# The expert stage's token tiles are turned by VectorE in one operation each, and the second tile's inner rows by TensorE

## The chip, the cores and the metric

One core of one Trainium2 chip. The metric is the device time of one execution in microseconds; the figure compared is the median of several runs. Lower is better.

## What is computed

All arrays are float32. The input of the expert layer comes from a small attention between 8x512 tokens and 8x32 state rows; its 4352 output rows of 512 columns go through eight experts and then a dense two-layer block:

```python
xread = softmax(x @ state.T / 8) @ state
sread = softmax(state @ x.T / 8) @ x
t = concatenate([xread, sread])            # 4352 rows of 512, heads side by side
e = argmax(t @ w_gate)                      # one expert per row, E = 8
h = maximum(t[e == i] @ w1[i], 0)           # 512 -> 1024
y = gate_weight * sigmoid(...) * (h @ w2[i])    # 1024 -> 512
u = y @ w_in                                # 512 -> 2048
g = where(u >= 1, u, where(u <= -1, 0, (u + 1)**2 / 4))
out = g @ w_out                             # 2048 -> 512
```

## The kernel before

The kernel has three stages. Every engine's instructions are written out by hand, each engine in its own program, and semaphores tie them together.

**Stage one (0 to about 150 us).** Eight steps, one for each batch, do the attention. The rows that come out are scattered to DRAM (`slot_x`) by GpSimd, sorted by expert. SP's queue loads the tokens of the next steps and, between them, the four units of the first expert's weights. A short passage at its end (VectorE's `choose`, `find`, `best_expert`, then the tables of tiles) works out which 128 rows make which tile and which expert each tile has. In this passage tiles 0 and 1 are already loaded and turned (`first_x`, `first_xs`).

**Stage two, the expert tiles (about 150 to 590 us).** There are 38 tiles of 128 rows, in a loop over t. A product needs its left operand with the contraction dimension on the partitions, so each tile's 128x512 rows are turned to `KD` = 4 blocks of 128x128, and the 128x1024 inner rows to `K1` = 8 blocks. A float32 value is split into a high part (rounded to the fast type) and a low part (the rest), and each product is three matmuls: high by high, high by low, low by high. For tile t:

- TensorE: `up(t)`, 24 matmuls of 512 columns (L1620), gives the inner rows of tile t in `pC`. `turn_x(t + 1)`, 4 transposes against the identity (L1554), turns the next tile's rows. `down(t - 1)`, 24 matmuls (L1665), gives the output of the tile before. So TensorE runs one tile behind itself: it does `up` of one tile while VectorE turns the inner rows of another.
- ScalarE: `relu(t)` to `hrow` (L723), `x_hi(t + 1)` (L700), the load of tile t + 2 to `xtile` (L719), `y_out(t - 1)` (L735, and its store L738), `h_hi(t)` in two halves (L729).
- VectorE: `turn_h(t)`, 16 transposes of 32x256, which turn the inner rows (L1220); after the first four of them `x_lo(t + 1)` (L1073); at the end `h_lo(t)` in two halves (L1230). `down(t)` waits for `hlo_done`, which the last of them raises.
- GpSimd splits the weights of the experts to come (L476, L478), four units each, and scatters the rows' places (L551). SP's queue loads those units to `stage` (L365).

VectorE's transpose works inside blocks of 32x32: element (i, j) of a block goes to (j, i) of a block, and a block stays in its group of 32 partitions unless the instruction's output is in another group. `turn_h` therefore issues one instruction for each pair of groups, 16 in all.

The order of TensorE's round is this piece of its program:

```python
def turn(t):
    up(t)
    turn_x(t + 1)
    down(t - 1)
```

Tile 1 is special: its inner rows are turned by `turn(1)` on VectorE, while tile 0's are turned by TensorE (`turn_first_h`, L1676), since VectorE is still busy with the tables then.

**Stage three (about 590 us to the end).** Nine blocks of rows go through the dense layers, with `hidden` (L1716) and `result` (L1730) on TensorE. Rows of the first blocks are already weighed and turned beside the last tiles of stage two (`turn_y`, L1702).

Of the kernel before, what the change touches and what calls it, by code (L numbers as in the profile page):

```python
# [30 lines left out]
P = 128  # L31
# [4 lines left out]
def build(nc, x, state, w_gate, w_ogate, w1, w2, w_in, w_out, out):  # L36
# [42 lines left out]
    with ctx:  # L79
# [251 lines left out]
        def rows_of(t):  # L331
            return xtile[:, :] if t is None else first_x[t][:, :]

        def quarter(e, q):
            return e % 2 * 2 + q // 2
# [16 lines left out]
        def _(sp):  # L352
# [15 lines left out]
            def expert_unit(e, q):  # L368
                if q < 2:
                    k = UNIT // F1  # L370
                    return w1[bass.ds(e, 1), q * k * P:(q + 1) * k * P, :].rearrange("o (k p) n -> p (o k) n", p=P)
                k = UNIT // DM
                return w2[bass.ds(e, 1), (q - 2) * k * P:(q - 1) * k * P, :].rearrange("o (k p) n -> p (o k) n", p=P)

# [7 lines left out]
            for b in range(2, B):  # L382
                load_x_next(b, b % 2)
                if b == 2:
                    for q in range(2):
                        load_unit(expert_unit(0, q), q)
                if b in (B - 3, B - 2):
                    q = 2 if b == B - 3 else 3
                    sp.wait_ge(weights_split, q - 1)
                    load_unit(expert_unit(0, q), q % 2)  # L390

            def load_expert(e, units):
                for q in units:
                    sp.wait_ge(weights_split, 4 * e + q - 1)
                    load_unit(expert_unit(e, q), q % 2)
# [48 lines left out]
        def _(pool):  # L444
# [25 lines left out]
            def split_unit(e, q, unit):  # L470

                at = W[:, bass.ds(quarter(e, q), 1), :, (q % 2) * UNIT:(q % 2 + 1) * UNIT]
                hi = at[:, :, HI, :].rearrange("p o n -> p (o n)")
                lo = at[:, :, LO, :].rearrange("p o n -> p (o n)")
                pool.wait_ge(stage_loaded[q % 2], 16 * (2 * e + q // 2 + 1))
# [51 lines left out]
            shift(B - 1, 1)  # L527
            pool.wait_ge(tile_loaded, 32)
            scatter(B - 3, 1)
# [43 lines left out]
            def next_expert(e):  # L573
# [6 lines left out]
                with pool.If(end < start + 1):  # L580
                    for q in range(4):
                        pool.wait_ge(stage_loaded[q % 2], 16 * (2 * e + q // 2 + 1))
# [28 lines left out]
        def _(act):  # L611
# [13 lines left out]
            def split_first(m, q):  # L625

                act.wait_ge(stage_loaded[q], 16 * m)
                hi = W[:, bass.ds(m - 1, 1), HI, q * UNIT:(q + 1) * UNIT].rearrange("p o n -> p (o n)")
# [125 lines left out]
            wait_for_rows()  # L754
            act.dma_start(xtile[:, :], slot_x[bass.ds(row, P), :]).then_inc(tile_loaded, 16)
            act.wait_ge(logit_shifted, 1)
# [121 lines left out]
        def _(dve):  # L878
# [354 lines left out]

            def turn(t, reuse=True):
                turn_h(t, 0, 1, reuse)
                x_lo(t + 1)
                turn_h(t, 1, 4)
                h_lo(t)

            slots_of_rows()  # L1240
            logits_of_rows()
            dve.wait_ge(hhi_done, 2)
            nc.vector.tensor_tensor(first_hs[:, LO, :, :], pD[:, :].rearrange("p (k s) -> p k s", k=K1),
                                    first_hs[:, HI, :, :].bitcast(F32), ALU.subtract).then_inc(hlo_done, 1)
# [73 lines left out]
            for a in range(2):  # L1318
                y_lo(a, 0, a)
            turn(tail + 1)  # L1320
            for a in range(2, BIG):
# [26 lines left out]
        def _(pe):  # L1348
# [200 lines left out]

            def turn_x(t, place=None):  # L1550
                pe.wait_ge(tile_loaded, 16 * (t + 1) if place is None else 32)
                turned, _ = x_at(place)
                for k in range(KD):
                    last = nc.tensor.transpose(turned[:, k * P:(k + 1) * P], rows_of(place)[:, k * P:(k + 1) * P], ident[:, :])  # L1554
                last.then_inc(xt_made, 1)
# [5 lines left out]
            turn_x(0, place=0)  # L1561
            pe.wait_ge(prob2_done, b + 1)
# [27 lines left out]
            pe.wait_ge(pT_copied, b + 1)  # L1590
            turn_x(1, place=1)
            pe.wait_ge(slots_found, r + 1)
# [42 lines left out]
            def up_first_two():  # L1635
# [9 lines left out]
                for n in range(2):  # L1645
                    pe.wait_ge(relu_done if n else relu_begun, 1)
                    if n:
                        turn_first_h()
                    for i in range(3 * KD):
# [21 lines left out]

            def turn_first_h():
                pe.wait_ge(relu_done, 1)
                pe.wait_ge(xread_copied[0], 2 * (B - 1) + CH)
                for k in range(K1):
                    last = nc.tensor.transpose(pD[:, k * P:(k + 1) * P], first_hrow[:, k * P:(k + 1) * P], ident[:, :])  # L1676
                last.then_inc(ht_made, 2)
# [114 lines left out]
```

## Time and profile before

| | us |
|---|---|
| median of 3 runs (1345.02 to 1346.15) | 1345.86 |
| the profiled execution, device time | 1341.72 |
| its span in the trace | 1339.70 |
| TensorE busy | 1318.6 (98%) |
| VectorE busy | 935.5 (70%) |
| ScalarE busy | 409.7 (31%) |
| GpSimd busy | 386.7 (29%) |

The span is the time from the first to the last instruction of the profiled execution; the device time holds what lies around it too. TensorE's busy time is modelled from the pipelined matmuls, so it tells that there is always one under way, not that each is as short as it could be. The chain of waits goes back from the last instruction to whatever released each step; what stands on it set the end. The granted TensorE clock is 0.996 of full speed over the span.

### The profile page before, as it was taken

To read this page: it belongs to the slowest core of one execution; us is meant where nothing else is said; L and a number is where in the kernel's file an instruction comes from. 1 tells how busy PE (TensorE), PEld (TensorE's weight loads), DVE (VectorE), ACT (ScalarE), POOL (GpSimd) and SP (SyncE) were. 2 spreads that over 40 slices of the span, in tenths; PEclk is the share of its full clock that TensorE was granted. 3 is DMA by queue.
4 is the path that set the end of the run, shared out by engine and by line. 5 is a ranking of instruction groups with operands and counts; after the bars stand their busy time and mean duration, and the time that the engine had idled before them with its cause. 6 is when DMAs were issued, how large, how long until landed. Compare 5 with 4: busy or idle time off the path is not lost.

```text
span 1339.7 us, 20092 instructions
## 1 busy us (share of the span) xinstructions
PE 1318.6 (98%) x6518; PEld 1104.4 (82%) x6519; DVE 935.5 (70%) x2001; ACT 409.7 (31%) x641; POOL 386.7 (29%) x213
## 2 busy tenths in 40 slices
PE   8999999999999999999999999999999999999996
PEld 6999888888888888887888888888888888888885
DVE  3667888888888888867777576675775767757343
ACT  3466322222222222322222222222222222222232
POOL 2377473876580939470010100100101001010010
PEclk9999999999999999999999999999999999999999
DMA  6556343534442425530010100100100001010000
GB/s 151 163 167 219 121 110 114 166 111 139 141 146 73 141 86 197 159 103 16 16 40 17 40 16 16 39 16 8 39 18 37 16 16 39 16 40 1 0 32 16
DMA packets 80589, 100.57 MB, mean 75 GB/s; under 512 B 46112, under 2 KB 46112, under 8 KB 80032
## 3 DMA queue, kind: packets, MB, share of 16 engines
q1 hardware_dynamic: 60160, 61.94, 15.3%
q10 hardware_dynamic: 13856, 20.19, 5.2%
q0 software_dynamic: 6528, 17.87, 3.5%
q8 instruction: 24, 0.39, 0.1%
q14 instruction: 21, 0.17, 0.0%
HBM read 69.80 MB, written 30.18 MB: 75 GB/s over the span
## 4 chain that ended last, share of the span: by engine, by line
PE 95%; DMA 1%; DVE 1%; ACT 1%; SPq 1%; ACTq 0%; issue 0%; POOL 0%; POOLq 0%; DVEq 0%
PE area L1716 27%; PE area L1730 27%; PE area L1665 16%; PE area L1620 15%; PE area L1430 2%; PE area L1400 2%; PE area L1420 1%; PE area L1554 1%; DMA xin<-in_x 1%; PE area L1387 1%; SPq L347 1%; PE area L1447 1%; DMA st_diag<-in_state 0%; PE area L1454 0%; DVE yrow L1259 0%
## 5 line engine op out<-in xcount | busy, mean ns | idle before, releaser
L1730 PE MATMUL area<-W,gs 128*128 128x512 f32 x1632 | 394.1, 389 | 1.8 <-DVE gs L1304 1.8
L1716 PE MATMUL area<-ys,W 128*128 128x512 f32 (+1 forms) x1728 | 394.3, 377 | 0.0
L1716 PEld LDWEIGHTS area<-ys,W 128*128 128x128 f32 x1728 | 313.4, 188 | 61.2
L1730 PEld LDWEIGHTS area<-W,gs 128*128 128x128 f32 x1632 | 305.2, 188 | 65.2 <-DVE gs L1304 2.6
L1220 DVE STREAM_TRANSPOSE area<-hrow 32x256 f32<-32x256 f32 x592 | 269.8, 456 | 74.5 <-ACT hrow L723 65.6
L605 POOL DMA_INDIRECT out<-orow,out_row x34 | 32.6, 960 | 695.0 <-ACT orow L811 606.4
L795 ACT ACTIVATE gate<-gate,half_col 128x512 f32<-128x512 f32 (+1 forms) x144 | 100.8, 700 | 379.5 <-DVE gate L1298 378.3
L1665 PE MATMUL area<-W,hs 128*128 x888 | 211.5, 394 | 0.0
L1298 DVE TENSOR_SCALAR gate<-area 128x512 f32<-128x512 f32 (+1 forms) x144 | 95.3, 662 | 156.8 <-PE area L1716 156.6
L1620 PE MATMUL area<-W,xs 128*128 x864 | 202.2, 390 | 0.0
L1665 PEld LDWEIGHTS area<-W,hs 128*128 128x128 f32 x888 | 164.1, 188 | 33.3 <-issue 0.2
L1620 PEld LDWEIGHTS area<-W,xs 128*128 128x128 f32 x864 | 162.0, 188 | 33.8 <-issue 0.3
L478 POOL TENSOR_TENSOR W<-stage,W 128x2048 fp32r<-128x2048 f32 x36 | 166.2, 4617 | 2.9
L1275 DVE STREAM_TRANSPOSE area<-yrow 32x128 f32<-32x128 f32 x480 | 154.7, 322 | 9.7
L1301 DVE TENSOR_TENSOR area<-gate,area 128x512 f32<-128x512 f32 (+1 forms) x144 | 96.0, 667 | 54.3 <-ACT gate L795 47.6
L1304 DVE TENSOR_TENSOR gs<-area,gs 128x512 fp32r<-128x512 f32 (+1 forms) x144 | 95.4, 662 | 36.1 <-ACT gs L802 32.1
L476 POOL CAST W<-stage 128x2048 fp32r<-128x2048 f32 x36 | 68.4, 1901 | 167.3 <-PE area L1620 145.5
L802 ACT CAST gs<-area 128x512 fp32r<-128x512 f32 (+1 forms) x144 | 81.1, 563 | 105.8 <-DVE area L1301 105.8
L735 ACT COPY ytile<-area 128x512 f32<-128x512 f32 x38 | 22.3, 587 | 165.0 <-PE area L1665 165.0
L729 ACT CAST hs<-area 128x512 fp32r<-128x512 f32 x74 | 43.5, 587 | 76.7 <-issue 43.3
L723 ACT ACTIVATE hrow<-area 128x1024 f32<-128x1024 f32 x37 | 38.0, 1027 | 56.2 <-PE area L1620 56.2
L1230 DVE TENSOR_TENSOR hs<-area,hs 128x512 fp32r<-128x512 f32 x74 | 48.6, 692 | 1.1
(198 smaller groups left out, 815.9 us busy)
## 6 DMA issues: line engine op xcount, KB each, us to landing
stage<-in_moe_w SPq DMA_DIRECT2D x32, 1024.0 KB, 5.6
sorted_y<-ytile ACTq DMA_DIRECT2D x38, 256.0 KB
xtile<-slot_x ACTq DMA_DIRECT2D x36, 256.0 KB, 2.7
yrow<-sorted_y SPq DMA_DIRECT2D x34, 256.0 KB, 2.7
xin<-in_x SPq DMA_DIRECT2D x60, 128.0 KB, 3.0
stage<-in_moe_w_in SPq DMA_DIRECT2D x4, 1024.0 KB, 5.4
stage<-in_moe_w_out SPq DMA_DIRECT2D x4, 1024.0 KB, 6.3
slot_x<-zero SPq DMA_DIRECT2D x9, 256.0 KB, 3.3
```

What stands on the lines that cost most here:

```text
L478: pool.tensor_tensor(lo, stage[:, q % 2, :], hi.bitcast(F32), ALU.subtract).then_inc(weights_split, 1)
L795: nc.scalar.activation(gate[n % 2][:, 0:width], gate[n % 2][:, 0:width], ACT.Square, bias=half_col[:, 0:1], scale=0.5).then_inc(squared, 1)
L802: nc.scalar.copy(gs[n % 2][:, HI, 0:width], HIDDEN[n % 2][:, 0:width]).then_inc(ghi_done, 1)
L1220: last = nc.vector.transpose(turned_rows(r // 2)[SQ * q:SQ * (q + 1), :, r % 2 * SQ:(r % 2 + 1) * SQ], hrow[SQ * r:SQ * (r + 1), :].rearra ...
L1275: last = nc.vector.transpose(turned[SQ * q:SQ * (q + 1), :, SQ * r:SQ * (r + 1)], yrow[k][SQ * r:SQ * (r + 1), :].rearrange("p (d f) -> p ...
L1298: nc.vector.tensor_scalar(g, h, -1.0, 1.0, ALU.max, ALU.min).then_inc(clamped, 1)
L1301: nc.vector.tensor_tensor(h, g, h, ALU.max).then_inc(gated, 1)
L1304: nc.vector.tensor_tensor(gs[n % 2][:, LO, 0:width], h, gs[n % 2][:, HI, 0:width].bitcast(F32), ALU.subtract).then_inc(glo_done, 1)
L1620: return nc.tensor.matmul(pC[:, n * NB:(n + 1) * NB], split[:, xp, k, :], W[:, bass.ds(e % 2 * 2, 1), wp, at:at + NB].rearrange("p o n -> ...
L1665: last = nc.tensor.matmul(pB[:, 0:NB], split[:, hp, k, :], W[:, bass.ds(e % 2 * 2 + 1, 1), wp, k * DM:(k + 1) * DM].rearrange("p o n -> p ...
L1716: last = nc.tensor.matmul(HIDDEN[n % 2][:, 0:width], wq[:, wp, :], ys[par][:, yp, k, 0:width], start=(k == 0 and wp == HI and yp == HI), s ...
L1730: last = nc.tensor.matmul(SUMS[a], gs[n % 2][:, gp, a * P:(a + 1) * P], W[:, q // 2 + 2, wp, at:at + DM], start=(n == 0 and gp == HI and w ...
```

## The change

Three things are changed.

1. **The rows of a tile are turned by one VectorE instruction.** `turn_x` moves from TensorE's program to VectorE's, where it is one transpose of 128x512 at the end of each round, for tile t + 2. Since the 32x32 blocks stay in their group of partitions, the rows have to come in another arrangement: `load_rows` issues four DMAs for a tile, one for each group of 32 partitions. Group q gets columns 128q to 128q + 127 of all 128 rows, four rows to a partition, in pieces of 512 bytes. After the transpose, partition 32q + s of block k holds column 128q + 32k + s.
2. **The first layer's weights come in the same order of rows.** The two units of `w1` are loaded by four DMAs each, of 32 partitions, instead of one of 128. `w2` is loaded as before. The counts that `stage_loaded` is waited for change with it (`unit_loaded`).
3. **The second tile's inner rows are turned by TensorE**: `turn_first_h(1, hrow)`, 8 transposes in the middle of `down(0)`, where `turn_x(2)` was; `turn(1)` leaves VectorE's program, and ScalarE takes the high parts of tile 1 in one copy ahead of `y_out(0)`.

```diff
+        def load_rows(engine, place, row):
+            for q in range(P // SQ):
+                engine.dma_start(rows_of(place)[SQ * q:SQ * (q + 1), :].rearrange("s (g c) -> s g c", c=P),
+                                 slot_x[bass.ds(row, P), P * q:P * (q + 1)].rearrange("(g s) c -> s g c", s=SQ)
+                                 ).then_inc(tile_loaded, 16)
...
             def expert_unit(e, q):
                 if q < 2:
                     k = UNIT // F1
-                    return w1[bass.ds(e, 1), q * k * P:(q + 1) * k * P, :].rearrange("o (k p) n -> p (o k) n", p=P)
+                    for part in range(P // SQ):
+                        at = P * part + SQ * k * q
+                        sp.dma_start(stage[SQ * part:SQ * (part + 1), q, :].rearrange("s (k n) -> s k n", k=k),
+                                     w1[bass.ds(e, 1), at:at + SQ * k, :].rearrange("o (k s) n -> s (o k) n", s=SQ)
+                                     ).then_inc(stage_loaded[q], 16)
...
             for t in range(2):
-                sp.dma_start(rows_of(t), slot_x[t * P:(t + 1) * P, :]).then_inc(tile_loaded, 16)
+                load_rows(sp, t, t * P)
...
-            pool.wait_ge(tile_loaded, 32)
+            pool.wait_ge(tile_loaded, 128)
...
             def load_tile(t):
                 row = act.value_load(tile_source[0:1, bass.ds(t, 1)], min_val=0, max_val=E * REGION - P)
-                act.dma_start(xtile[:, :], slot_x[bass.ds(row, P), :]).then_inc(tile_loaded, 16)
+                load_rows(act, None, row)
...
             load_tile(3)
+            act.wait_ge(ht_made, 4)
+            nc.scalar.copy(hs[:, HI, :, :], pD[:, :].rearrange("p (k s) -> p k s", k=K1)).then_inc(hhi_done, 2)
             y_out(0, first_two=True)
-            h_hi(1)
...
+            def turn_x(t, place=None):
+                dve.wait_ge(tile_loaded, 64 * (t + 1) if place is None else 128)
+                if place is None:
+                    dve.wait_ge(xlo_done, t)
+                turned, _ = x_at(place)
+                nc.vector.transpose(turned.rearrange("p (k g s) -> p k g s", k=KD, s=SQ),
+                                    rows_of(place).rearrange("p (g k s) -> p k g s", k=KD, s=SQ)).then_inc(xt_made, 1)
...
+            dve.wait_ge(col_exp, B)
+            turn_x(0, place=0)
             read_out(r, 0, 3, None)
...
             find(r, 0, CH, ROUTE * r + 6, LAST_RANKS)
+            dve.wait_ge(pT_copied, B)
+            turn_x(1, place=1)
...
-            def turn(t, reuse=True):
-                turn_h(t, 0, 1, reuse)
+            def turn(t, last=False):
+                turn_h(t, 0, 1)
                 x_lo(t + 1)
                 turn_h(t, 1, 4)
                 h_lo(t)
+                if not last:
+                    turn_x(t + 2)
...
             places_of_tiles()
-            turn(1)
+            turn_x(2)
             weights_of_rows()
+            x_lo(2)
+            first_h_lo(1, hs)
+            turn_x(3)
...
-            down(0, True, between=lambda: turn_x(2))
+            down(0, True, between=lambda: turn_first_h(1, hrow))
...
             def turn(t):
                 up(t)
-                turn_x(t + 1)
                 down(t - 1)
```

TensorE's program at the seam between `up(t)` and `down(t - 1)`, in the loop over the tiles, before the change:

```order
L1620 MATMUL area<-W,xs 128x512 x3
L1551 ISA
L1554 MATMUL area<-ident,xtile 128x128 [waits tile_loaded]
L1554 MATMUL area<-ident,xtile 128x128 x3
L1615 ISA
L1615 TENSOR_LOAD tile_expert
L1615 ISA x2
L1657 ISA
L1665 ISA [waits y_copied,hlo_done,weights_split]
L1665 MATMUL area<-W,hs 128x512
```

And after it (line numbers are those of the changed kernel):

```order
L1651 MATMUL area<-W,xs 128x512 x3
L1646 ISA
L1646 TENSOR_LOAD tile_expert
L1646 ISA x2
L1688 ISA
L1696 ISA [waits y_copied,hlo_done,weights_split]
L1696 MATMUL area<-W,hs 128x512
```

The four transposes and their wait are gone, and the instruction that waits for `hlo_done` stands right behind the last matmuls of `up`.

VectorE's program at the end of a round, in its loop over the tiles, after the change:

```order
L1101 TENSOR_TENSOR xs<-area,xs 128x512 [waits xhi_done]
L1252 STREAM_TRANSPOSE area<-hrow 32x8x32 x12
L1260 ISA
L1262 TENSOR_TENSOR hs<-area,hs 128x8x64 [waits hhi_done]
L1260 REGISTER_ALU
L1262 TENSOR_TENSOR hs<-area,hs 128x8x64 [waits hhi_done]
L1091 ISA
L1095 STREAM_TRANSPOSE area<-xtile 128x512 [waits xlo_done,tile_loaded]
L1288 REGISTER_ALU
L1288 COMPARE_AND_BRANCH
```

The rows down to the second TENSOR_TENSOR were there before; the ISA and the transpose of 128x512 behind them are new, ahead of the jump back to the next tile's `turn_h`.

## Rows read from the trace of the kernel before

**Rows 1.** The page's head and its first part: the span, TensorE's busy time.

```profile
span 1339.7 us, 20092 instructions
PE 1318.6 (98%) x6518; PEld 1104.4 (82%) x6519; DVE 935.5 (70%) x2001; ACT 409.7 (31%) x641; POOL 386.7 (29%) x213
```

**Rows 2.** Chain of waits, tile stage; start us, us, what.

```profile
401.03 0.44 PE area L1554 x4
401.47 5.46 PE area L1665 x24
406.93 5.44 PE area L1620 x24
```

**Rows 3.** Chain of waits, first and last rounds of the stage.

```profile
174.06 5.73 PE area L1665 x24
179.80 5.44 PE area L1620 x24
...
543.21 5.44 PE area L1620 x24
...
567.91 5.49 PE area L1620 x24
```

**Rows 4.** Timeline of VectorE, one round; start us, us, what, idle before.

```profile
402.13 1.86 DVE L1220 STREAM_TRANSPOSE area<-hrow 32x256 f32<-32x256 f32 x4 [1.92 <-ACT hrow L723]
403.90 0.67 DVE L1073 TENSOR_TENSOR xs<-area,xs 128x512 fp32r<-128x512 f32 x1
404.60 5.64 DVE L1220 STREAM_TRANSPOSE area<-hrow 32x256 f32<-32x256 f32 x12
410.27 1.31 DVE L1230 TENSOR_TENSOR hs<-area,hs 128x512 fp32r<-128x512 f32 x2
```

**Rows 5.** Timeline of ScalarE and its queue, the same round.

```profile
401.07 1.03 ACT L723 ACTIVATE hrow<-area 128x1024 f32<-128x1024 f32 x1 [1.58 <-PE area L1620]
...
402.26 0.34 ACTq L719 DMA_DIRECT2D xtile<-slot_x  x1
```

**Rows 6.** Timeline of weight loads (PEld) and of VectorE, two places.

```profile
406.55 5.40 PEld L1620 LDWEIGHTS area<-W,xs 128*128 128x128 f32 x24
...
172.46 1.31 DVE L1230 TENSOR_TENSOR hs<-area,hs 128x512 fp32r<-128x512 f32 x2
...
174.04 0.99 PEld L1665 LDWEIGHTS area<-W,hs 128*128 128x128 f32 x5 [0.22 <-issue]
```

**Rows 7.** Three VectorE lines (ns min/median/max) and, from the page's fifth part, GpSimd's split.

```profile
L1220 DVE STREAM_TRANSPOSE area<-hrow x592: 441/457/468, 163.8 to 581.6; 32x256 f32<-32x256 f32 x198
...
L1275 DVE STREAM_TRANSPOSE area<-yrow x480: 306/324/334, 605.3 to 1231.3; 32x128 f32<-32x128 f32 x160
...
L1259 DVE TENSOR_SCALAR yrow<-yrow,info_of x30: 476/486/4671, 598.6 to 1215.3; 128x512 f32<-128x512 f32 x30
...
L478 POOL TENSOR_TENSOR W<-stage,W 128x2048 fp32r<-128x2048 f32 x36 | 166.2, 4617 | 2.9
```

**Rows 8.** Timeline ahead of the tile stage.

```profile
133.98 1.06 PE L1439 MATMUL area<-ident,prob2T 128*128 128x128 f32 x8 [0.29 <-ACT rows L622]
...
142.91 0.19 DVE L1088 COPY record_now<-area 128x32 f32<-128x32 f32 x1 [1.23 <-PE area L1581]
```

**Rows 9.** Queues of SP, GpSimd and ScalarE; the last row is the page's sixth part.

```profile
38.60 1.13 SPq L365 DMA_DIRECT2D stage<-in_moe_w  x2
48.77 36.89 SPq L347 DMA_DIRECT2D xin<-in_x  x24
...
124.15 0.43 SPq L400 DMA_DIRECT2D first_x<-slot_x  x1
...
132.46 1.11 POOL L504 DMA_INDIRECT slot_x<-rows,found  x1 [1.75 <-DVE found L931]
...
160.32 0.39 ACTq L755 DMA_DIRECT2D xtile<-slot_x  x1
...
xtile<-slot_x ACTq DMA_DIRECT2D x36, 256.0 KB, 2.7
```

More of the change, by code:

```diff
@@ L332, in rows_of, with unit_loaded @@
             return xtile[:, :] if t is None else first_x[t][:, :]
+        def load_rows(engine, place, row):
[3 more added lines that the diff above has]
+                                 ).then_inc(tile_loaded, 16)
+        def unit_loaded(e, q):
+            if e < E:
+                return 80 * e + (64 if q < 2 else 80)
+            return 80 * E + 32 * (e - E) + 16 * (q // 2 + 1)
         def quarter(e, q):
@@ L370, in expert_unit @@
                     k = UNIT // F1
-                    return w1[bass.ds(e, 1), q * k * P:(q + 1) * k * P, :].rearrange("o (k p) n -> p (o k) n", p=P)
-                k = UNIT // DM
-                return w2[bass.ds(e, 1), (q - 2) * k * P:(q - 1) * k * P, :].rearrange("o (k p) n -> p (o k) n", p=P)
+                    for part in range(P // SQ):
[3 more added lines that the diff above has]
+                                     ).then_inc(stage_loaded[q], 16)
+                else:
+                    k = UNIT // DM
+                    load_unit(w2[bass.ds(e, 1), (q - 2) * k * P:(q - 1) * k * P, :].rearrange("o (k p) n -> p (o k) n", p=P), q % 2)
             def load_x_next(b, par):
@@ L385, in _ @@
                     for q in range(2):
-                        load_unit(expert_unit(0, q), q)
+                        expert_unit(0, q)
                 if b in (B - 3, B - 2):
@@ L389, in _ @@
                     sp.wait_ge(weights_split, q - 1)
-                    load_unit(expert_unit(0, q), q % 2)
+                    expert_unit(0, q)
             def load_expert(e, units):
@@ L394, in load_expert @@
                     sp.wait_ge(weights_split, 4 * e + q - 1)
-                    load_unit(expert_unit(e, q), q % 2)
+                    expert_unit(e, q)
             for par in range(2):
@@ L474, in split_unit @@
                 lo = at[:, :, LO, :].rearrange("p o n -> p (o n)")
-                pool.wait_ge(stage_loaded[q % 2], 16 * (2 * e + q // 2 + 1))
+                pool.wait_ge(stage_loaded[q % 2], unit_loaded(e, q))
                 pool.tensor_copy(hi, stage[:, q % 2, :]).then_inc(hi_split, 1)
@@ L581, in next_expert @@
                     for q in range(4):
-                        pool.wait_ge(stage_loaded[q % 2], 16 * (2 * e + q // 2 + 1))
+                        pool.wait_ge(stage_loaded[q % 2], unit_loaded(e, q))
                         pool.wait_ge(weights_split, 4 * e + q)
@@ L625, in split_first @@
             def split_first(m, q):
-                act.wait_ge(stage_loaded[q], 16 * m)
+                act.wait_ge(stage_loaded[q], 16 * m + 48)
                 hi = W[:, bass.ds(m - 1, 1), HI, q * UNIT:(q + 1) * UNIT].rearrange("p o n -> p (o n)")
@@ L754, in _ @@
             wait_for_rows()
-            act.dma_start(xtile[:, :], slot_x[bass.ds(row, P), :]).then_inc(tile_loaded, 16)
+            load_rows(act, None, row)
             act.wait_ge(logit_shifted, 1)
@@ L1238, in turn, with first_h_lo @@
                 h_lo(t)
+                if not last:
+                    turn_x(t + 2)
+            def first_h_lo(t, split):
+                dve.wait_ge(hhi_done, 2 * t + 2)
+                nc.vector.tensor_tensor(split[:, LO, :, :], pD[:, :].rearrange("p (k s) -> p k s", k=K1),
+                                        split[:, HI, :, :].bitcast(F32), ALU.subtract).then_inc(hlo_done, 1)
             slots_of_rows()
             logits_of_rows()
-            dve.wait_ge(hhi_done, 2)
-            nc.vector.tensor_tensor(first_hs[:, LO, :, :], pD[:, :].rearrange("p (k s) -> p k s", k=K1),
-                                    first_hs[:, HI, :, :].bitcast(F32), ALU.subtract).then_inc(hlo_done, 1)
+            first_h_lo(0, first_hs)
             places_of_tiles()
-            turn(1)
+            turn_x(2)
             weights_of_rows()
+            x_lo(2)
+            first_h_lo(1, hs)
+            turn_x(3)
             with dve.Fori(2, TT - 2) as t:
@@ L1319, in _ @@
                 y_lo(a, 0, a)
-            turn(tail + 1)
+            turn(tail + 1, last=True)
             for a in range(2, BIG):
@@ L1548, in _ @@
                     step(2 * m + par, par)
[L1550 to L1555, printed above, removed]
             b, r = B - 1, B - 2
@@ L1560, in _ @@
             nc.tensor.matmul(FIRST_COUNT, ones[:, :], tally[1][:, 0:2], start=True, stop=True).then_inc(first_rows_made, 1)
-            turn_x(0, place=0)
             pe.wait_ge(prob2_done, b + 1)
@@ L1590, in _ @@
             pe.wait_ge(pT_copied, b + 1)
-            turn_x(1, place=1)
             pe.wait_ge(slots_found, r + 1)
@@ L1647, in up_first_two @@
                     if n:
-                        turn_first_h()
+                        turn_first_h(0, first_hrow)
                     for i in range(3 * KD):
@@ L1670, in down, with turn_first_h @@
                 last.then_inc(down_done, 1)
-            def turn_first_h():
-                pe.wait_ge(relu_done, 1)
-                pe.wait_ge(xread_copied[0], 2 * (B - 1) + CH)
+            def turn_first_h(t, of):
+                pe.wait_ge(relu_done, t + 1)
+                if t == 0:
+                    pe.wait_ge(xread_copied[0], 2 * (B - 1) + CH)
                 for k in range(K1):
-                    last = nc.tensor.transpose(pD[:, k * P:(k + 1) * P], first_hrow[:, k * P:(k + 1) * P], ident[:, :])
+                    last = nc.tensor.transpose(pD[:, k * P:(k + 1) * P], of[:, k * P:(k + 1) * P], ident[:, :])
                 last.then_inc(ht_made, 2)
```

## The prediction

> **What bounds the kernel now.** I read the page's first part: TensorE is busy for 98% of the span [rows 1]. That alone says little, since its busy time is modelled, so the next view is the chain of waits. Through the whole tile stage it runs on TensorE only, and one round reads: 4 transposes 0.44 us, 24 matmuls of `down` 5.46, 24 of `up` 5.44, then the next transposes [rows 2]. So a round is 5.44 / 24 = 0.227 us for each matmul and half a microsecond for the transposes, and nothing in it waits. From the `up` at 179.80 to the one at 543.21 there are 32 rounds in 363.41 us, 11.36 each [rows 3]. Two `up` and `down` of 5.44 without the transposes would take 10.88; the 0.48 between is what the change can win in a round on TensorE: 0.44 of transposes and 0.02 to 0.05 in the `down` behind them.
>
> The second thing to read is what hides beside it. The timeline of VectorE shows one round: four transposes from 402.13, `x_lo`, twelve transposes, `h_lo` to 410.27 + 1.31 = 411.58; ahead of the first of them it was idle for 1.9 us behind `relu` [rows 4]. That is 9.45 us of work without a gap. ScalarE's `relu` starts at 401.07, 0.04 behind the end of `up` at 401.03 [rows 2, 5]. So from the end of `up(t)` to the end of `h_lo(t)` it takes 411.58 - 401.03 = 10.55 us, and `down(t)` needs that before it can start. Now `down(t)` starts one round behind the `down` at 401.47 [rows 2], at 412.8, 1.2 us later than `h_lo` ends, so nobody waits. This chain is what the change comes close to.
>
> **The change part by part.**
>
> *The moved transpose on VectorE.* The trace has no transpose over 128 partitions. A 32x256 one takes 0.457 us and a 32x128 one 0.324, so 128 more elements in a partition cost 0.133; 512 elements then take 0.457 + 2 x 0.133 = 0.72 us, if the four groups of partitions go through together [rows 7]. If they go one after another it is 4 x 0.72 = 2.9. I take 0.72, because every other VectorE instruction of the round works on 128 partitions by 512 elements in 0.67 to 0.69 [rows 4]. The Trainium skill (Vector Engine (DVE) Microarchitecture Reference, section 3.8) has the reordering array in front of each 32-channel bank and lets it sustain one element per cycle per lane, which would be the first price; no row here shows an instruction that could prove it. In the round it stands behind `h_lo`, so it delays nothing of tile t; the next `turn_h` waits for `relu` anyway. Of the 1.9 us idle, the faster round takes 0.35 and this 0.72, which leaves 0.8. Cost: none, covered by the idle time in front of `turn_h`; without that cover 0.72 a round.
>
> *Its rows.* Four DMAs by 0.34 us of ScalarE's queue instead of one [rows 5]: from 402.26 the issue ends near 403.7, or 405 if each needs as long as SP's two in 1.13 [rows 9]. ScalarE's next work, `y_out`, waits for `down` to end, 5.44 behind 401.03, at 406.5. The last piece lands 2.7 us behind its issue [rows 9], by 408, and VectorE wants it at 411.6. Cost: none.
>
> *The chain that now binds.* With the transposes gone, `down(t)` would follow `up(t + 1)` at 401.03 + 10.88 = 411.91. TensorE loads the first weights of a group 0.38 ahead of its place in the chain (406.55 against 406.93) [rows 2, 6], so it wants them at 411.53. `h_lo` ends at 411.58, and there is a place that shows how long the wake-up takes: at the first round `h_lo` ends at 172.46 + 1.31 = 173.77 and the weight load of `down(1)` begins at 174.04 [rows 6], 0.27 later, with an idle time of 0.22 that is put down to issue (behind the waiting instruction stand register work and the matmul, in the same order now as before). So the load would start at 411.85, 0.32 late. From a load that waited to the end of `down` it is 174.06 + 5.73 - 174.04 = 5.75 us [rows 3]; one that didn't wait takes 0.38 + 5.44 = 5.82. The loss is 0.32 - 0.07 = 0.25 us, but only every other time: two rounds last 10.55 + 0.27 + 5.75 + 5.44 = 22.01, since the tile in between starts its chain early against its `down`. A round is 11.01 us. The ends of the unknown wake-up are 0 and 0.27 or more: with no wait at all the round is 10.88. I take 0.27, the one row there is. Each further 0.1 us in the chain costs 0.05 a round, 1.6 us in all.
>
> *The sum.* The 32 rounds: 32 x (11.36 - 11.01) = 11.1 us. The first round: `down(1)` loses its transposes and its wait for `h_lo`, since TensorE now turns tile 1's rows and VectorE's 7.5 us of `turn_h(1)` are gone: (0.44 + 5.73) - 5.44 = 0.7 us. The two rounds at the end, which also turn rows of stage three, lie at 543.21 to 567.91, 24.70 us; one loses 0.35, the other, whose chain has more room, 0.5: 0.9 us. Together 12.7.
>
> *Ahead of the stage.* `turn_x(0)` on TensorE lay in a gap (its next matmul was idle for 0.29 behind ScalarE) [rows 8]: nothing won. On VectorE 0.72 us stand ahead of `read_out`, where 0.5 was idle; the rest is taken up before the next wait for TensorE. `turn_x(1)` stands in a VectorE gap of 1.23 us [rows 8]: 0.44 won on TensorE. The 8 transposes in `down(0)` in place of 4: 0.44 lost. Tile 2 is the tight spot: its DMAs are issued from 160.32 on [rows 9], four by 0.39, landing by about 164.5; transpose 165.2, weights 166.9, `x_lo(2)` 167.6, and TensorE wants it with 0.27 of wake-up at 167.8. Even; up to 1 us lost if the load is slower. Together 0.
>
> *SP's queue.* Six more DMAs behind 38.60 at 0.57 end at 43.2, before the token loads at 48.77. The eight pieces of tiles 0 and 1 begin 0.4 ahead of 124.15 and, at 0.43 to 0.57 each and 2.7 to land, are there by 130 to 131; GpSimd's scatter, which waits for them, goes at 132.46 [rows 9]. For the experts, `w1`'s six extra issues an expert stand in a queue that waits for GpSimd. None on the path.
>
> The profiled execution then takes 1341.72 - 12.7 = 1329.0 us. It was 4.1 us below the median of the runs, and I lay the gain against the median: 1345.86 - 12.7 = **1333.2 us**.
>
> **The rivals.**
>
> *No wait.* If the wake-up is short enough, the round is 10.88, and the 32 rounds win 15.4; with the rest 17.0 us: 1328.9. For it: most waits in this trace end with an idle time far below 0.22. Against it: `h_lo` ends 0.05 behind the moment at which the load is wanted, so some wait is nearly sure.
>
> *A longer chain.* ScalarE's extra issues, SP's and ScalarE's DMAs or a slower tile 2 could stretch the 10.55 by up to the 0.35 that a round still has over the old one, half of which is lost: 32 x 0.18 = 5.6, giving 7.1 of gain: 1338.8. Nothing in VectorE's order inside the chain changes, which speaks against it.
>
> *GpSimd's port.* One VectorE instruction that reads and writes on-chip rows, L1259, took 4.67 us in place of 0.49, beside a split of GpSimd's (L478, 4.62 us, 36 times in 420 us, 39% of the time) [rows 7]. If the new transpose is held up in the same way, then in 39% of the rounds it waits 2.3 us on average, 1.5 beyond the 0.8 of room: 32 x 0.39 x 1.5 = 19 us, half to all of it lost: 1343 to 1352. Against it: the 592 transposes of `turn_h` read the same kind of rows, ran beside the same splits and never took over 0.468 [rows 7]. The Trainium skill (SBUF — State Buffer, section on who interferes with whom) lets only VectorE operations in two-port modes or with two SBUF inputs contend with GpSimd; the 0.468 agrees.
>
> *VectorE becomes the bound (slower).* The four groups go one after another, 2.9 us: a round of VectorE is 9.45 + 2.9 + 0.05 = 12.4, 1.04 over the old one, and 33 rounds lose 34 us: 1380. It decides from a transpose of 11.36 - 9.45 = 1.9 us up. Only that the trace has no such form speaks for it.
>
> **How the numbers follow.** Late `h_lo` as computed 0.50 (its own range 1331.5 to 1335), no wait 0.22, longer chain 0.17, GpSimd's port 0.06 (half of it slower), VectorE the bound 0.05. The range goes from just below the no-wait case to just above the longer chain, 1328.3 to 1339.5. Faster or slower is meant by over 0.2%, 2.7 us, which is about what a measurement of this kernel can tell from no change. Faster 0.90; same 0.03; slower 0.07.
>
> **What would show it.** Right: no TensorE transposes against `xtile`; one VectorE transpose of 128x512 near 0.72 us behind `h_lo`; rounds in the chain that alternate near 10.9 and 11.1, 22.0 for two; a wait of TensorE's weight loads for `h_lo` or issue of about 0.3 in every second round; first `up` of the loop where it was, near 168.2. Wrong: all rounds at 10.88 (wake-up overrated), a transpose over 1.9 us, or one whose longest is near 5 us (port), or `turn_h` waiting for something other than `relu`.

## The result, and the profile after

| | us |
|---|---|
| before, median of 4 runs (1345.02 to 1347.41) | 1346.01 |
| after, median of 4 runs (1333.31 to 1333.72) | 1333.53 |
| ratio | 0.9906 [0.9889, 0.9924] |
| profiled execution after, device time | 1333.59 |

The changed kernel is 12.5 us faster, with an interval of 10.2 to 14.9. The prediction was 1333.2 us and a gain of 12.7. The page's head and first part, of after:

```profile
span 1331.5 us, 20311 instructions
...
PE 1305.4 (98%) x6374; PEld 1088.9 (82%) x6375; DVE 955.6 (72%) x2022; ACT 410.5 (31%) x640; POOL 387.2 (29%) x213
```

Against [rows 1], TensorE has 144 matmul records fewer (38 times 4 transposes of rows gone, 8 of tile 1's inner rows new) and 13.2 us less of busy time; VectorE has 20 us more. TensorE still fills 98% of the span, so the engine that bounds the kernel is the same and each round of it is shorter. The chain of waits of after, first rounds of the stage (start us, us, what):

```profile
173.11 5.44 PE area L1651 x24
178.55 5.44 PE area L1696 x24
183.99 5.44 PE area L1651 x24
189.43 5.68 PE area L1696 x24
195.11 5.45 PE area L1651 x24
200.56 5.45 PE area L1696 x24
```

The 0.44 of [rows 2] between `up` and `down` is gone. The `down` at 189.43 takes 5.68 where its neighbours take 5.44 or 5.45; the next at 211.45 takes 5.65. From 189.43 to 211.45 are two rounds, 22.02 us. The whole stretch of [rows 3] and the two rounds behind it read, in the same view:

```profile
536.15 5.44 PE area L1651 x24
541.59 5.52 PE area L1696 x24
547.10 0.87 PE area L1733 x8
...
559.75 5.46 PE area L1651 x24
```

From 183.99 to 536.15 the 32 rounds last 352.16 us, 11.00 each (363.41 before); the last two last 23.60 (24.70 before). Where the 5.68 comes from stands in the timeline of VectorE, ScalarE and the weight loads, one round of after (start us, us, what, idle before):

```profile
387.59 1.03 ACT L741 ACTIVATE hrow<-area 128x1024 f32<-128x1024 f32 x1 [1.27 <-PE area L1651]
388.57 1.78 ACTq L337 DMA_DIRECT2D xtile<-slot_x  x4
388.65 1.86 DVE L1252 STREAM_TRANSPOSE area<-hrow 32x256 f32<-32x256 f32 x4 [0.85 <-ACT hrow L741]
...
396.79 1.31 DVE L1262 TENSOR_TENSOR hs<-area,hs 128x512 fp32r<-128x512 f32 x2
...
398.13 0.73 DVE L1095 STREAM_TRANSPOSE area<-xtile 128x512 f32<-128x512 f32 x1
398.37 1.66 PEld L1696 LDWEIGHTS area<-W,hs 128*128 128x128 f32 x8 [0.33 <-issue]
```

`relu` starts at 387.59, 0.04 behind the end of `up`, and `h_lo` ends at 396.79 + 1.31 = 398.10: 10.55 us, the number that was read from [rows 4, 5]. The first weight load of `down` follows at 398.37, 0.27 later, and sat idle for 0.33. The `down` behind it waits too, for 0.18. The same waits summed over the stage by the view of waits (engine and line waited for: us in total, times, longest):

```profile
409.27 4.84 PEld L1696 LDWEIGHTS area<-W,hs 128*128 128x128 f32 x22 [0.18 <-issue]
...
PEld area L1696 <- issue: 7.5, 29, 0.4
```

So 29 of the 37 `down`s from `down(1)` on wait, not every second one. In all 29 the load begins 0.26 to 0.30 us behind the end of `h_lo`. The picture of a long and a short `down` holds only for the first rounds; in the middle of the stage the chain of waits reads:

```profile
310.51 5.57 PE area L1696 x24
...
321.52 5.55 PE area L1696 x24
...
332.51 5.58 PE area L1696 x24
```

Two rounds still last 332.51 - 310.51 = 22.00 us. The reason is in the order of the work: `up(t + 2)` follows `down(t)`, and `down(t)` waits for the chain that began at the end of `up(t)`. The chain therefore fixes the distance of two rounds. How the 22.0 us divide between the two, it leaves open, as long as neither is under 10.88: at first they are 10.88 and 11.13, later 11.00 and 11.00.

The moved transpose stands behind `h_lo` and costs 0.73; the idle time ahead of the next `turn_h` is 0.85 where it was 1.92 [rows 4]. VectorE's lines (ns min/median/max), and GpSimd's split from the page's fifth part, which answers to [rows 7]:

```profile
L1095 DVE STREAM_TRANSPOSE area<-xtile x36: 718/727/728, 168.3 to 552.2; 128x512 f32<-128x512 f32 x36
...
L1299 DVE TENSOR_SCALAR yrow<-yrow,info_of x30: 475/486/4649, 590.4 to 1207.1; 128x512 f32<-128x512 f32 x30
...
L496 POOL TENSOR_TENSOR W<-stage,W 128x2048 fp32r<-128x2048 f32 x36 | 166.3, 4619 | 2.9
```

All 36 transposes take 0.718 to 0.728 us. L1299 (L1259 before) has its one long execution as it had.

One row does not fit: the first `up` of the loop starts at 173.11, not at 168.19 as before. The first experiment asks why.

### The profile page after: what moved, and what is told of

Read it like the earlier page. It is cut to its first block, busy times and chain, and to the rows that moved or that the text cites. A ratio compares the mean times of both kernels' runs of the same rounds, so it can differ in the third digit from the quotient of the medians.

```text
span 1331.5 us, 20311 instructions
## 1 busy us (share of the span) xinstructions
PE 1305.4 (98%) x6374; PEld 1088.9 (82%) x6375; DVE 955.6 (72%) x2022; ACT 410.5 (31%) x640; POOL 387.2 (29%) x213
## 4 chain that ended last, share of the span: by engine, by line
PE 93%; DVE 2%; ACT 1%; issue 1%; DMA 1%; SPq 1%; another core or an unknown queue 0%; POOL 0%; POOLq 0%; DVEq 0%; ACTq 0%
PE area L1747 27%; PE area L1761 27%; PE area L1696 16%; PE area L1651 16%; PE area L1470 2%; PE area L1440 1%; PE area L1460 1%; DMA xin<-in_x 1%; PE area L1427 1%; PE area L1487 1%; SPq L360 1%; PE area L1494 0%; DVE rowsum L1036 0%; DVE yrow L1299 0%
## 5 line engine op out<-in xcount | busy, mean ns | idle before, releaser
L1252 DVE STREAM_TRANSPOSE area<-hrow 32x256 f32<-32x256 f32 x576 | 262.6, 456 | 41.4 <-ACT hrow L741 32.1
```

The source lines that it names most:

```text
L1252: last = nc.vector.transpose(turned_rows(r // 2)[SQ * q:SQ * (q + 1), :, r % 2 * SQ:(r % 2 + 1) * SQ], hrow[SQ * r:SQ * (r + 1), :].rearra ...
```

## The experiments

Twelve kernels ran, four each in three jobs; every time below is set against runs of the kernel before in its own job. The line numbers in a fence are those of its own kernel, a few lines off from one kernel to the next.

**1 and 2. Both kernels again, side by side.** No edit.

> The kernel before, unchanged, profiled once more. Its first profile took 1341.72 us and reached the first up of the tile loop at 168.19 us; its other executions took 1345.0 to 1347.4. Theory A (the token loads of the first stage are slower by some 4 us in most executions, whatever the kernel): 1345 to 1346, first up at 172 to 173, steps of the first stage 0.8 us longer each. Theory B (the change itself costs the 4.9 us by which its profile reached the loop later): first up near 168.2 again and the remaining 4 us of the executions somewhere behind it.

> The changed kernel, unchanged, once more on the same chip as the others. Both theories: 1333.5, two rounds of the tile loop in 22.0 us, first up of the loop at 173.1.

Measured: before again 1341.26 (ratio 1.0005 [0.9995, 1.0015]), after again 1328.51, ratio 0.9915 [0.9898, 0.9931]. Neither expectation came: both kernels were some 5 us faster than in the first job, and both reached the first `up` of the loop early. Chains of waits, before again and then after again:

```profile
149.57 8.43 PE area L1620 x36
...
167.65 5.44 PE area L1620 x24
...
173.53 5.73 PE area L1665 x24
179.26 5.44 PE area L1620 x24
```

```profile
148.64 8.43 PE area L1651 x36
...
167.11 5.44 PE area L1651 x24
...
177.99 5.44 PE area L1651 x24
183.43 5.68 PE area L1696 x24
```

The kernel before took 1346.0 us in the first job and 1340.6, 1341.0 and 1344.4 in the next three, so a whole job is shifted by up to 5 us, for both kernels alike. The last three jobs ran on three different chips, so whether the shift belongs to the job or to the chip is not shown. It lies ahead of the tile stage: the changed kernel's first `up` comes 6.00 us earlier here than in the first job, and its span is 6.1 us shorter; the 32 rounds of the kernel before are 363.41 us in both of its traces so far. The late 173.11 is therefore not due to the change; side by side the changed kernel's first `up` is 0.54 us earlier. The kernel before had its 168.19 in a profiled execution that was 4 us faster than its other runs. This pair gives the account of the gain: 0.54 ahead of the stage, 11.61 - 10.88 = 0.73 in the first round, 363.41 - 352.00 = 11.41 in the 32 rounds, 1.26 in the last two, together 13.9 against 14.0 between the spans (1339.4 and 1325.4). The medians of the runs differ by 12.1.

**3 and 4. The weights' order by itself.** In the kernel before, `w1`'s units are loaded by four DMAs each, in their old order of rows; in the changed kernel they are loaded whole again (its rows of `w1` then don't stand in the order of the tile's columns).

```diff
+                    for part in range(P // SQ):
+                        sp.dma_start(stage[SQ * part:SQ * (part + 1), q, :].rearrange("s (k n) -> s k n", k=k),
+                                     src[SQ * part:SQ * (part + 1), :, :]).then_inc(stage_loaded[q], 16)
```

> The kernel before with each w1 unit loaded by four DMAs of 32 partitions, rows in their old order. Theory A (loads of w1 in pieces lie beside other work): within 0.5 us of the kernel before in this job. Theory B (the six extra issues on SP's queue in the first stage, or their traffic, hold up the token loads): 2 to 5 us slower, first up at 170 to 173.

> The changed kernel with w1 loaded by one DMA for each unit as before, so that the first layer's product uses weights' rows in an order that does not fit the turned rows (the output is not the reference's). Theory A: 1333.5, as the changed kernel. Theory B (pieces of w1 cost the first stage): 1329 to 1331, first up near 168.5.

Measured: 1341.41, ratio 1.0007 [0.9997, 1.0016], and 1328.31, ratio 0.9907 [0.989, 0.9923]. SP's queue in the kernel before with the pieces, beside [rows 9]:

```profile
37.15 3.91 SPq L379 DMA_DIRECT2D stage<-in_moe_w  x8
47.26 6.37 SPq L353 DMA_DIRECT2D xin<-in_x  x8
```

Eight issues take 3.91 us in place of 1.13 for two and end at 41.1, 6 us ahead of the next token loads. Run 3 is 0.8 us over the kernel before and 0.15 over run 1, which is the same kernel; run 4 is 0.2 under run 2. The pieces cost nothing that can be measured, in either kernel.

**5 and 6. A longer and a shorter chain.** One more turn of 32x256 in each `turn_h`, into a spare buffer; and one turn fewer (one block of 32 partitions of the inner rows is not turned).

```diff
+                    if r == 2:
+                        nc.vector.transpose(spare[0:SQ, :].rearrange("p (k s) -> p k s", k=K1),
+                                            hrow[SQ * r:SQ * (r + 1), :].rearrange("p (k f) -> p k f", k=K1)[:, :, 0:SQ])
```

```diff
-                    for q in range(4):
+                    for q in range(4) if r != 2 else (0, 1, 3):
```

> The changed kernel with one more transpose of 32x256 in each round's turning of inner rows (its output goes to a spare buffer), about 0.47 us in the chain from relu to h_lo. Theory A (the chain from the end of up(t) to down(t) binds in every second round, so half of what it grows is lost): two rounds last 22.0 + 0.47 = 22.5 us, the 32 rounds 7.5 us more than in the changed kernel. Theory B (VectorE's time is still hidden and the 11.0 us round is TensorE's own pace): no difference. Theory C (the chain is lost in full every round): 15 us more.

> The changed kernel with one of the 16 transposes of 32x256 left out of each round (one block of the inner rows isn't turned, so the second layer works on the tile before's). The chain is 0.47 us shorter. Theory A: h_lo is early by 0.15 us, nothing waits, a round is 2 x 5.44 = 10.88 us and two are 21.76; 32 rounds take 4.0 us less than in the changed kernel. Theory B: no difference. Theory C: 8 us less.

Measured: 1335.74, ratio 0.9961 [0.9946, 0.9975], and 1324.53, ratio 0.9878 [0.9861, 0.9894]. Against their own job's before (1340.97) these are -5.2 and -16.4 us, where the changed kernel had -12.1: 6.8 longer and 4.4 shorter. The chain of waits with one turn more:

```profile
185.02 0.40 issue
185.42 5.71 PE area L1700 x24
...
207.46 0.40 issue
207.85 5.73 PE area L1700 x24
```

The wait is now long enough to stand in the chain by itself, in every second round (the weight loads wait in 30), and two rounds last 207.46 - 185.02 = 22.44 us. Its 32 rounds take 539.24 - 179.59 = 359.65, which is 7.65 more than 352.00. From 185.02 to the issue at 521.76 are fifteen pairs of rounds, 22.45 us each: 0.45 more than 22.00, the turn's 0.46 once for two rounds. The sixteenth is 22.92; a round ahead of it VectorE's moved transpose had waited 0.59 us for the load of its tile. With one turn less every piece is 5.44, TensorE waits nowhere in the stage, and the 32 rounds take 527.35 - 179.19 = 348.16 = 32 x 10.88. So the chain through `h_lo` binds, half of what is put into it is paid, and 3.84 us is all that it costs in the changed kernel.

**7. The moved transpose twice.** A second transpose of 128x512 from `xtile`, into a spare buffer, ahead of the real one.

```diff
+                if place is None:
+                    nc.vector.transpose(spare[:, :].rearrange("p (k g s) -> p k g s", k=KD, s=SQ),
+                                        rows_of(place).rearrange("p (g k s) -> p k g s", k=KD, s=SQ))
```

> The changed kernel with the 128x512 transpose of each tile issued twice (the first one's output goes to a spare buffer), both behind h_lo: 0.73 us more of VectorE in a round, outside the chain. In the trace VectorE is idle for 0.69 and 0.85 us in alternate rounds ahead of the next turning. Theory A (only the chain counts, this is idle time): within 1.5 us of the changed kernel. Theory B (VectorE is the bound of the round now): 0.73 a round, 23 us more.

Measured: 1331.37, ratio 0.9928 [0.9911, 0.9944], 2.5 us over the changed kernel. That is under neither expectation. The timeline of VectorE, two rounds:

```profile
394.49 0.70 DVE L1097 STREAM_TRANSPOSE spare<-xtile 128x512 f32<-128x512 f32 x1
395.21 0.73 DVE L1099 STREAM_TRANSPOSE area<-xtile 128x512 f32<-128x512 f32 x1
395.84 1.82 DVE L1256 STREAM_TRANSPOSE area<-hrow 32x256 f32<-32x256 f32 x4
...
407.10 1.86 DVE L1256 STREAM_TRANSPOSE area<-hrow 32x256 f32<-32x256 f32 x4 [0.48 <-ACT hrow L742]
```

In one of two rounds `turn_h` follows at once, in the other after 0.48: the room behind `h_lo` is just used up, as 0.8 of room against 0.70 of work says. It takes 31 rounds 342.35 us where the changed kernel has 341.05, 1.3 more. About 1.1 of the 1.3 falls on two places. Two rounds take 22.5 us there in place of 22.0, each time a round behind a transpose that had to wait for its tile's rows, once for 0.71 us and once for 0.92:

```profile
383.80 0.71 DVE L1097 STREAM_TRANSPOSE spare<-xtile 128x512 f32<-128x512 f32 x1 [0.92 <-DMA xtile<-slot_x]
```

In the other rounds two stay at 21.97 to 22.08, so the second transpose fits where the load is in time. The rest is one place near the end of the stage, in the chain of waits, where ScalarE's queue issued a piece of a tile for 1.58 us and the weighing of `yrow` stood behind it:

```profile
541.43 1.58 ACTq L338
...
543.11 0.73 ACT yrow L846
```

The four issues there took 3.16 us together, against 1.86 at the same place of run 2. What held the one back is not shown. So the room in VectorE's round holds a second transpose, but nothing beyond it: a load that comes late, or a slow issue, then reaches TensorE. In run 2 no transpose waited for a load.

**8. Waiting later for the low parts.** `down` waits for `hhi_done` at its start, and for `hlo_done` at its third matmul, which is the first that reads the low parts.

```diff
-                pe.wait_ge(hlo_done, t + 1)
+                pe.wait_ge(hhi_done, 2 * t + 2)
...
                     for hp, wp in ((HI, HI), (HI, LO), (LO, HI)):
+                        if k == 0 and hp == LO:
+                            pe.wait_ge(hlo_done, t + 1)
```

> The changed kernel, but down(t) waits for the high parts (hhi_done) ahead of its first matmul and for the low parts (hlo_done) only ahead of its third, the first that reads a low part. High parts are ready 0.7 us before the low ones. Theory A (the wait for h_lo and its wake-up cost 0.25 us in every second round): rounds of 10.88 us, 32 x 0.125 = 4.0 us less than the changed kernel, the weight loads' waits for issue gone. Theory B (the seam between up and down costs this whatever is waited for): no difference.

Measured: 1324.19, ratio 0.9879 [0.9863, 0.9896]. The interval lies below that of the changed kernel (0.9898 to 0.9931), so this version beats both, though by little and from another job (the first job's 0.9889 to 0.9924 overlaps it; the traces below decide it). Its chain of waits:

```profile
183.97 5.44 PE area L1698 x24
...
194.85 5.44 PE area L1698 x24
```

Every `down` of the 32 rounds is 5.44 and every round 10.88; they take 348.16 us, the same as with a turn less. This is the "no wait" case of the prediction, brought about by 0.45 us of later need.

**9. The third part alone.** In the kernel before, tile 1's inner rows are turned by TensorE in the middle of `down(0)`; the tile rows stay on TensorE.

```diff
-            turn(1)
+            x_lo(2)
...
-            down(0, True, between=lambda: turn_x(2))
+            def between():
+                turn_x(2)
+                turn_first_h(1, hrow)
```

> The kernel before with the third part of the change alone: tile 1's inner rows are turned by TensorE in the middle of down(0), beside the transposes of the rows, which stay on TensorE. Theory A (the late h_lo is the only large term): the eight transposes add 0.87 us to down(0), the wait of down(1) for h_lo (0.27) goes, and VectorE has turned rows that nobody waits for earlier; so the time is that of the kernel before within 1 us, most likely 0.6 longer, and the chain of waits shows down(1) at 5.46 in place of 5.73. Rival: this part carries a share of the gain of its own, because VectorE's passage of choose, find and tables gets 7.5 us of turn_h less: then at least 2 us shorter.

Measured: 1346.26 beside 1344.36, ratio 1.0015 [1.0006, 1.0025]: 1.9 us longer, between 0.8 and 3.4; the 0.6 expected lies just outside. The rival is out. Its chain of waits:

```profile
167.92 0.87 PE area L1681 x8
...
171.57 5.44 PE area L1624 x24
...
177.45 5.46 PE area L1669 x24
...
558.80 1.44 issue
```

The 0.87 is there and `down(1)` takes 5.46 in place of 5.73, as expected: 0.6. Another 1.44 us of issue stands inside an `up` at the end of the stage. Run 1 has 0.19 us of it at 556.54, run 10 has 1.02 at 558.89, and in the first trace of the kernel before a weight load sat idle for 0.29 there. All are kernels of the old round; no chain of the changed kernel has it. What it is, and whether the change or chance removed it, stays open.

**10. The later wait, in the kernel before.** The edit of run 8 in the old round.

> The kernel before with the wait for the low parts moved from the start of down to its third matmul. Theory A (the wait costs only where h_lo comes after TensorE wants it): in this kernel h_lo ends 1.2 us ahead of down, so nothing changes in a round; the one wait of down(1) goes: same time within 0.5 us, rounds at 11.36. Rival (the order of register work and waits at the start of down costs something by itself): every round gets shorter by 0.1 or more, over 3 us in all.

Measured: 1344.68, ratio 1.0002 [0.9992, 1.0011]. Its 32 rounds last 545.25 - 181.84 = 363.41 us, to the hundredth those of the kernel before. The edit that wins 4 to 5 us in the changed kernel is worth nothing where `h_lo` is 1.2 us early: the wait it moves was created by the change.

**11. Each tile in one load.** The four DMAs of `load_rows` become one of 128x512 in plain order; the columns then don't stand in the order of the weights' rows.

```diff
-            for q in range(P // SQ):
-                engine.dma_start(rows_of(place)[SQ * q:SQ * (q + 1), :].rearrange("s (g c) -> s g c", c=P),
...
+            engine.dma_start(rows_of(place), slot_x[bass.ds(row, P), :]).then_inc(tile_loaded, 16)
```

> The changed kernel with each tile's rows loaded by one DMA of 128x512 in plain order; the columns then don't stand in the order of the weights' rows, so the products are of other numbers, the work is the same. Theory A (the four DMAs and their issues cost nothing): the time of the changed kernel, 1328.5, within 1 us, a ratio near 0.991. Rival (three more issues on ScalarE and on SP, or pieces of 512 bytes, cost something): 1326.5 or less.

Measured: 1332.68, ratio 0.992 [0.9904, 0.9937]; the changed kernel's 0.9915 would be 1332.9 in this job. ScalarE's queue:

```profile
387.43 0.34 ACTq L336 DMA_DIRECT2D xtile<-slot_x  x1
```

One issue of 0.34 us in place of 1.78 for four changes nothing: its 32 rounds take 534.81 - 182.82 = 351.99 us.

**12. One turn more and the later wait together.** The edits of runs 5 and 8.

> The changed kernel with the wait for the low parts at the third matmul of down and one more turn of 32x256 (0.46 us) in each turn_h. Alone, the first gave 1324.2 and the second 1335.7. Theory A (the later wait gives the chain 0.45 us more time, no more): two rounds last 10.55 + 0.46 + 0.27 + 5.75 - 0.45 + 5.44 = 22.02 with a wake-up of 0.27, and 21.9 with one of 0.15, where 21.76 is the least: 16 x 0.14 to 16 x 0.26 over 1324.2, 1326.4 to 1328.4. Rival (the later wait won for another reason, and the turn costs its 7.2 as before): 1331.4. Second rival (the wait no longer binds at all): 1324.2.

Measured: 1329.53, ratio 0.9887 [0.9871, 0.9904]. Its 32 rounds take 532.75 - 183.39 = 349.36 us: 1.2 over run 8, 10.3 under run 5. Both rivals are out: the turn that cost 7.65 us with the early wait costs 1.2 with the late one. (By the medians, each against its own job, the turn costs 2.0.) Theory A's mechanism holds, but it expected 2.2 to 4.2. The timeline of VectorE, ScalarE and the weight loads shows why, in the round with the longest wait:

```profile
385.93 0.73 DVE L1096 STREAM_TRANSPOSE area<-xtile 128x512 f32<-128x512 f32 x1 [0.70 <-DMA xtile<-slot_x]
...
395.12 1.32 DVE L1266 TENSOR_TENSOR hs<-area,hs 128x512 fp32r<-128x512 f32 x2
...
395.13 0.59 ACT L748 CAST hs<-area 128x512 fp32r<-128x512 f32 x1 [1.98 <-DVE area L1256]
...
395.92 0.32 PEld L1702 LDWEIGHTS area<-W,hs 128*128 128x128 f32 x2 [0.32 <-issue]
396.50 4.90 PEld L1702 LDWEIGHTS area<-W,hs 128*128 128x128 f32 x22 [0.25 <-DVE hs L1266]
```

`h_lo` ends at 396.44 and the load that waits for it begins at 396.50, 0.06 later; in the three other rounds in which the weight loads wait for `h_lo` it is 0.05, 0.05 and 0.06. In run 2 the wait at the start of `down` needed 0.27. With 0.06 in theory A's sum two rounds last 21.81 us, and 349.36 / 16 = 21.84 were measured. The round shown is not a usual one: its `down` takes 5.79 us where all others of the loop take 5.44 to 5.52. VectorE's transpose ahead of it had waited 0.70 us for the load of its tile, so the whole chain was late, and here alone the high parts bind too: ScalarE's cast ends at 395.72 and the first load begins at 395.92.

## Why the prediction was right, point by point

**The round.** "11.36, at least 10.88": both were found, 363.41 / 32 before and 348.16 / 32 in runs 6 and 8.

**The moved transpose.** Forecast 0.72 us, measured 0.727, all four groups of partitions together. The sentence on the reordering array (the Trainium skill, Vector Engine (DVE) Microarchitecture Reference, section 3.8) now has a row: L1095 agrees with groups that go side by side, and excludes 2.9. "Cost: none, leaves 0.8": the idle time is 0.69 to 0.85 in the rounds read, and run 7 shows that it holds a second one.

**Its rows.** Forecast four issues of 0.34, none on the path; they took 1.78 together, done at 404.0 by the forecast's clock, between its 403.7 and 405, and run 11 shows that they cost nothing. The 2.7 us from issue to landing was too low as a bound: in runs 5, 7 and 12 the transpose waited for its rows one, two and four times, up to 0.92 us. In both traces of the changed kernel itself it never did, so the term was nothing as forecast, with less room than the sum shows.

**The chain.** This was the step that carried the number. The 10.55 stayed 10.55, the wake-up of 0.27 was 0.26 to 0.30 in all 29 waits, two rounds of 22.01 were 22.0 all through the loop. One detail was wrong and cost nothing: "only every other time". So was the sign of rounds that alternate near 10.9 and 11.1, but for the first ones. The waits fall in 29 of 37 `down`s, at about half the length where both of a pair wait, and only their sum over two rounds is fixed. Run 5 shows that what is added to the chain is paid once in two rounds, as "each further 0.1 us costs 0.05 a round" had it; runs 6 and 8 give back 3.84 us, where 4.2 lie between rounds of 11.01 and 10.88. 11.1 us was forecast for the 32 rounds, 11.41 measured (11.25 in the first job's profile; the forecast without its rounding is 363.41 - 16 x 22.01 = 11.25 as well).

**First and last rounds.** 0.7 forecast, 0.73 measured. The last two: 0.9 forecast, 1.1 measured against [rows 3] (24.70 - 23.60); the 5.64 there held 0.2 of issue, which I had not looked into. By the pair of run 1 and run 2 it is 1.26, and the 0.19 of issue at 556.54 is part of that, so some 0.2 of the total may not be due to the change.

**Ahead of the stage.** "Together 0" was the loosest term, and 0.54 was won. `up(0)` starts 0.93 earlier, about half of it the 0.44 of `turn_x(1)`, the rest already gained before it, where I had put nothing for `turn_x(0)`; `down(0)` with its eight transposes is 0.39 longer and takes as much back. Tile 2 was no tight spot: its `x_lo` ends at 165.1 in run 2 and TensorE wants it at 167.1.

**The other queues.** Forecast none, and runs 3 and 4 show none.

**The sum.** 12.7 forecast; 12.5 [10.2, 14.9] and 12.1 [9.3, 13.7] measured, and 13.9 by the pair of profiles. The terms were each slightly low. That the value fell within 0.4 us of the median owes something to the choice to lay the gain against the runs' median and not against the profiled execution, which was 4 us faster than the runs beside it.

**The rivals.** *No wait* did not come by itself, and is what run 8 makes. *A longer chain*: the 10.55 did not grow. *GpSimd's port*: none of the 36 transposes was over 0.728 us, beside splits of 4.62. The rule that was weighed there (the Trainium skill, SBUF — State Buffer, section on who interferes with whom) agrees with that 0.728; the 4649 ns of L1299 is another matter. It starts at 590.45, 0.24 us behind the start of a split of 4.61 us, and ends 0.28 behind the split's end; in the kernel before it is the same with 0.22 and 0.28. That looks like an instruction held out by the split, but no run moved either of them, so it is not shown. *VectorE becomes the bound*: 0.727 against 1.9.

## What to carry to other kernels

Taking work off the engine that bounds a loop shortens it only down to the next dependency cycle: add up the durations from the end of one product to the start of the one that needs it, and compare with the new round, wake-up included. If the work is pipelined over two tiles, such a cycle spans two rounds, and then half of each saving or cost in it counts for a round. Read it from the length of two rounds, not from the wait of one: the wait moves between the two, the sum doesn't. When it is late by a few tenths, look for what the waiting instruction needs first: moving a wait behind two matmuls that don't need the data won as much here as taking a transpose out of the chain.

## What the runs showed of the hardware that was not expected

- **The same wait costs TensorE 0.27 us or 0.06, by where it stands.** At the start of `down`, on an instruction with register work and a matmul behind it, the load came 0.26 to 0.30 us behind the end of `h_lo`, in all 29 waits of the changed kernel's first trace; at the third matmul it came 0.05 to 0.06 behind, in all four waits of run 12. Which part of the 0.21 the register work has was not measured.
- **A job, or the chip it ran on, shifts both kernels by up to 5 us, nearly all of it ahead of the tile stage**: the kernel before took 1340.6 to 1346.0 us in four jobs, and its 32 rounds took 363.41 us in all five traces of the old round.
- **An issue on a hardware queue is not always 0.34 us.** One on ScalarE's queue took 1.58 (run 7), and behind it stood work of the engine itself.
- **A load of 256 KB does not always land 2.7 us behind its issue.** In run 7 the four pieces of a tile were issued by 374.14 + 1.78 = 375.92, with a load of 1 MB of weights issued at 374.80 beside them, and the transpose that waited for them began at 383.80, 7.9 us later. That the weights held them up is likely, but no run took them away.
